# A routing stage rewritten: slot table by float16 products, probabilities after it, counts ahead of the prefix product, last gate by halves

## The reference

```
logits = einsum('bsd,de->bse', x, w_gate)
local_gate = 1 / (1 + exp(-einsum('bsd,de->bse', x, w_local)))
for b, s:
    fresh_e = argmax(logits[b, s])
    e = fresh_e if s == 0 or local_gate[b, s] < 0.5 else prev_e
    prev_e = e
    p = softmax(logits[b, s])            # the sum has 1e-9 added
    h = relu(x[b, s] @ w1[e])            # 512 -> 1024
    out[b, s] = p[e] * (h @ w2[e])       # 1024 -> 512
```

## Time and profile before

| | |
|---|---|
| median of three runs | 1024.58 us (1024.54 to 1025.24) |
| the profiled execution's own time | 1025.83 us |
| its span from the first to the last instruction | 1023.7 us |
| busy in the span: PE, DVE, ACT, POOL | 92%, 45%, 35%, 25% |
| the last tile's second product ends | at 665.4 us |
| first product of the expert blocks starts | at 711.0 us |

### The profile page before, as it was taken

One profiled execution on the slowest core, in us unless ns is written; L12 is line 12 of the kernel. 1 busy time (PEld: TensorE's weight loads), 2 busy tenths in 40 slices (PEclk: granted clock), 3 DMA queues, 4 the chain that ended last, 5 costly groups with the idle time before them and its releaser, 6 DMA issues.

```text
span 1023.7 us, 20276 instructions
## 1 busy us (share of the span) xinstructions
PE 940.4 (92%) x7890; PEld 613.2 (60%) x7891; DVE 458.1 (45%) x830; ACT 356.0 (35%) x472; POOL 254.1 (25%) x265
## 2 busy tenths in 40 slices
PE   4899997999999999999999999915899999999995
PEld 2566665787767677676777676603455555555552
DVE  4688885465334242433333343558924786000000
ACT  2677774443111111121221111010444454454442
POOL 2345543110101010110202000001334444334331
PEclk9999998999999999999999999956899999999998
DMA  8243441433101110101101102403734664111100
GB/s 300 83 137 122 138 125 40 137 104 118 55 28 35 41 41 20 41 20 41 41 20 41 41 11 98 139 23 131 234 91 162 197 210 150 41 38 40 46 25 1
DMA packets 50812, 87.18 MB, mean 85 GB/s; under 512 B 6069, under 2 KB 21636, under 8 KB 50510
## 3 DMA queue, kind: packets, MB, share of 16 engines
q1 hardware_dynamic: 45325, 70.52, 21.6%
q0 software_dynamic: 5440, 16.00, 5.0%
HBM read 71.78 MB, written 16.55 MB: 86 GB/s over the span
## 4 chain that ended last, share of the span: by engine, by line
PE 86%; DVE 8%; issue 2%; DMA 1%; ACT 1%; POOL 1%; DVEq 0%; SPq 0%; POOLq 0%; ACTq 0%
PE psum L743 18%; PE psum L758 18%; PE psum L891 13%; PE psum L867 12%; PE psum L688 6%; PE psum L543 5%; PE psum L700 2%; PE psum L880 2%; DVE m_mem L1146 2%; DVE arena L1174 2%; PE psum L855 1%; PE psum L564 1%; PE psum L598 1%; PE psum L617 1%; PE psum L718 1%
## 5 line engine op out<-in xcount | busy, mean ns | idle before, releaser
L743 PE MATMUL psum<-m_mem,arena 128*128 (+1 forms) x1728 | 198.8, 273 | 0.3 <-DVE arena L1376 0.3
L758 PE MATMUL psum<-arena,m_mem 128*128 128x512 f16 x864 | 195.3, 379 | 0.0
L743 PEld LDWEIGHTS psum<-m_mem,arena 128*128 128x128 f16 x1728 | 168.3, 98 | 26.0 <-DVE arena L1376 0.6
L758 PEld LDWEIGHTS psum<-arena,m_mem 128*128 128x128 f16 x864 | 84.5, 98 | 90.4
L867 PE MATMUL psum<-arena,m_mem 128*128 x600 | 137.0, 386 | 1.4 <-ACT m_mem L1077 1.4
L891 PE MATMUL psum<-arena,m_mem 128*128 x600 | 133.6, 379 | 2.3 <-ACT m_mem L1091 2.3
L1022 ACT ACTIVATE m_mem<-psum 128x512 f16<-128x512 f32 x72 | 43.0, 597 | 257.8 <-PE psum L743 255.8
L867 PEld LDWEIGHTS psum<-arena,m_mem 128*128 128x128 f16 x600 | 58.7, 99 | 69.0 <-issue 5.9
L1292 DVE SCALAR_TENSOR_TENSOR m_mem<-psum,m_mem 128x512 f16<-128x512 f32 x72 | 49.8, 691 | 111.6 <-ACT m_mem L1022 109.6
L891 PEld LDWEIGHTS psum<-arena,m_mem 128*128 128x128 f16 x600 | 57.7, 98 | 67.5 <-issue 2.4
L1574 POOL TENSOR_TENSOR arena<-m_mem,arena 128x1024 f16<-128x1024 f32 x9 | 17.9, 1994 | 264.7 <-ACT arena L1032 264.7
(11 more groups left out here) (198 smaller groups left out, 1147.8 us busy)
## 6 DMA issues: line engine op xcount, KB each, us to landing
dimdft_sb<-in_exp_w SPq DMA_DIRECT2D x74, 256.0 KB, 3.2
wstage<-in_exp_w SPq DMA_DIRECT2D x54, 256.0 KB, 2.8
m_mem<-in_qk SPq DMA_DIRECT2D x16, 576.0 KB, 4.7
arena<-in_v SPq DMA_DIRECT2D x32, 160.0 KB, 4.3
x_rows<-m_mem SPq DMA_DIRECT2D x16, 320.0 KB, 3.1
x_rows<-arena SPq DMA_DIRECT2D x9, 512.0 KB, 2.8
wstage<-in_mlp_w SPq DMA_DIRECT2D x16, 256.0 KB, 2.7
arena<-in_mlp_w SPq DMA_DIRECT2D x16, 256.0 KB, 2.7
```

What stands on the lines that cost most here:

```text
L743: last = nc.tensor.matmul(psum[:, 2 + k % 4, (f % 2) * 2 * P:(f % 2 + 1) * 2 * P], w1_sb[:, sp_, c, f * P:(f + 1) * P], unT[:, bass.ds(t % ...
L758: last = nc.tensor.matmul(psum[:, 6 + q, :], hT[:, k % 4, sp_, at:at + P], w2_sb[:, mp, f, :], start=f == 0 and sp_ == 0 and mp == 0, stop ...
```

## The change

Four edits.

1. **Last gate by halves.** Behind the last tile, the 256 rows go through transpose, high part, low part and gate in two halves of 128 rows, each with its own semaphore. `x2_done` is now raised by DVE behind the second low part. DVE also subtracts one prefix matrix from the other there.
2. **Running counts ahead.** `onehot` is made directly from PSUM, and DVE scans it along the groups (`ocum`) before the product. The product of the triangle less the ones with `onehot`, plus that of the ones with `ocum`, gives the position within the expert; an extra product of 8 columns gives the totals. The copies to `ef`, `tot` and the two additions into `before` are gone, and `psel` runs behind the scan.
3. **Slots on partitions, in float16.** `onehot_slot` becomes the weights, in float16, and `row_vals` (row number less 1152) the moving side with 25 columns, so the table's first column comes out in place. Its one consumer, the gather of block 0, starts from it directly, without POOL's copy. 
4. **The rest afterwards.** The expert of each block, the three bfloat16 parts of the probability (`p_part`, `p_vals`), the tokens (`tok_vals`), and 36 more products on PE follow behind `table_ready`, and the other table columns, seven small instructions, behind those (`rest_ready`). On PE the 36 products stand ahead of `transpose_xe(0)`. Four small DVE instructions (a float16 copy of the place numbers, the offset ids) are added where DVE waits for the DRAM transfer.

```diff
@@ end of the last tile, PE
-            transpose_x2(MT - 1)
-            gate(MT - 1)
+            for q in range(2):
+                pe.wait_ge(end_x2, q + 1)
+                for c in range(DC):
+                    last = nc.tensor.transpose(psum[:, q, c * P:(c + 1) * P], x2_sb[:, q, c * P:(c + 1) * P],
+                                               ident_sb[:, :])
+                last.then_inc(end_turned, 1)
+            for q in range(2):
+                pe.wait_ge(end_lo, q + 1)
+                last = gate_half(q)
+            last.then_inc(gate_ready, 1)
@@ end of the last tile, ACT
-            x2T_copy(MT - 1)
+            for q in range(2):
+                act.wait_ge(end_turned, q + 1)
+                nc.scalar.activation(x2T[:, 0, q], psum[:, q, :], ACT.Copy).then_inc(end_hi, 1)
             x2_hi_of(MT - 1)
@@ end of the last tile, DVE
-            x2T_lo_of(MT - 1)
+            x2_of(MT - 1, False, end=True)
+            dve.wait_ge(tables_in, 9 * 16)
+            nc.vector.tensor_tensor(prefix_sb[:, 0, :], prefix_sb[:, 0, :], prefix_sb[:, 1, :], ALU.subtract)\
+                .then_inc(parts_ready, 1)
+            for q in range(2):
+                dve.wait_ge(end_hi, q + 1)
+                nc.vector.tensor_tensor(x2T[:, 1, q], psum[:, q, :], x2T[:, 0, q], ALU.subtract).then_inc(end_lo, 1)
+            dve.wait_ge(end_x2, 2)
+            dve.sem_inc(x2_done, 1)
             logits_of(MT - 1)
@@ counts and slot table, PE
-            nc.tensor.matmul(psum[:, 3, 0:E * NT], prefix_sb[:, 1, :], flat1h, start=True, stop=True)
-            nc.tensor.matmul(psum[:, 4, 0:E * NT], prefix_sb[:, 0, :], flat1h, start=True, stop=True)\
+            pe.wait_ge(parts_ready, 1)
+            nc.tensor.matmul(psum[:, 4, 0:E * NT], prefix_sb[:, 0, :], flat1h, start=True, stop=False)
+            pe.wait_ge(onehot_ready, 2)
+            nc.tensor.matmul(psum[:, 3, 0:E], prefix_sb[:, 1, :], ocum[:, :, NT - 1], start=True, stop=True)
+            nc.tensor.matmul(psum[:, 4, 0:E * NT], prefix_sb[:, 1, :], ocum.rearrange("p e n -> p (e n)"), start=False, stop=True)\
                 .then_inc(counts_ready, 1)
             for n in range(NT):
                 pe.wait_ge(rec_ready, n + 2)
-                last = nc.tensor.matmul(psum[0:3 * NBLK, 5, 0:P], slot_vals[:, n].rearrange("p w k -> p (w k)"),
-                                        onehot_slot[:, n, :], start=n == 0, stop=n == NT - 1)
+                last = nc.tensor.matmul(psum[:, 5, 0:NBLK], onehot_slot[:, n, :], row_vals[:, n, :],
+                                        start=n == 0, stop=n == NT - 1)
             last.then_inc(slots_ready, 1)
-            pe.wait_ge(slots_copied, 1)
-            nc.tensor.transpose(psum[:, 6, 0:3 * NBLK], slotsT[0:3 * NBLK, :], ident_sb[0:3 * NBLK, 0:3 * NBLK])\
-                .then_inc(slots_ready, 1)
+            pe.wait_ge(vals_ready, 1)
+            for n in range(NT):
+                nc.tensor.matmul(psum[:, 1, 0:NBLK], onehot_slot[:, n, :], tok_vals[:, n, :],
+                                 start=n == 0, stop=n == NT - 1)
+                last = nc.tensor.matmul(psum[:, 7, 0:3 * NBLK], onehot_slot[:, n, :],
+                                        p_vals[:, n].rearrange("p w k -> p (w k)"), start=n == 0, stop=n == NT - 1)
+            last.then_inc(slots_ready, 1)
@@ counts, DVE
-            step(nc.vector.tensor_copy(ef, psum[:, 2, 0:NT]))
-            step(nc.vector.tensor_tensor(onehot, iota_sb, bc(ef, E, 1), ALU.is_equal))
-            nc.vector.tensor_tensor(psel, onehot, pex.rearrange("p n e -> p e n"), ALU.mult)\
+            nc.vector.tensor_tensor(onehot, iota_sb, bc(psum[:, 2, 0:NT], E, 1), ALU.is_equal).then_inc(onehot_ready, 1)
+            dve.wait_ge(onehot_ready, 1)
+            nc.vector.tensor_tensor_scan(fl(ocum), fl(reset_sb), fl(onehot), 0.0, ALU.mult, ALU.add)\
                 .then_inc(onehot_ready, 1)
+            step(nc.vector.tensor_tensor(psel, onehot, pex.rearrange("p n e -> p e n"), ALU.mult))
             dve.wait_ge(counts_ready, 1)
-            step(nc.vector.tensor_copy(tot, psum[:, 3, 0:E * NT].rearrange("p (e n) -> p e n", e=E)))
-            step(nc.vector.tensor_tensor_scan(fl(run), fl(reset_sb), fl(tot), 0.0, ALU.mult, ALU.add))
-            step(nc.vector.tensor_tensor(over, bc(run[:, :, NT - 1], NT, 2), thr_sb, ALU.is_gt))
+            step(nc.vector.tensor_tensor(over, bc(psum[:, 3, 0:E], NT, 2), thr_sb, ALU.is_gt))
...
-            step(nc.vector.tensor_tensor(before, run, tot, ALU.subtract))
-            step(nc.vector.tensor_tensor(before, before, bc(start, NT, 2), ALU.add))
@@ slot table, DVE
-            step(nc.vector.tensor_copy(posf2, posi))
-            nc.vector.tensor_reduce(psl, psel.rearrange("p e n -> p n e"), AX.X, ALU.add)
-            step(nc.vector.tensor_tensor(isblk, blk_iota, bc(posf2[:, 1, :], NBLK, 2), ALU.is_equal))
-            nc.vector.tensor_tensor(slot_vals[:, :, 0, :], isblk, bc(ids_sb[:, 0, :], NBLK, 2), ALU.mult)
-            nc.vector.tensor_tensor(slot_vals[:, :, 1, :], isblk, bc(ids_sb[:, 1, :], NBLK, 2), ALU.mult)
-            nc.vector.tensor_tensor(slot_vals[:, :, 2, :], isblk, bc(psl, NBLK, 2), ALU.mult).then_inc(rec_ready, 1)
+            nc.vector.tensor_copy(posf2, posi[:, 0, :])
+            step(nc.vector.tensor_tensor(isblk, blk_iota, bc(posi[:, 1, :], NBLK, 2), ALU.is_equal))
+            nc.vector.tensor_tensor(row_vals, isblk, bc(id_vals[:, 0, :], NBLK, 2), ALU.mult).then_inc(rec_ready, 1)
             for n in range(NT):
-                nc.vector.tensor_scalar(onehot_slot[:, n, :], slot_iota, posf2[:, 0, n:n + 1], None, ALU.is_equal)\
+                nc.vector.tensor_scalar(onehot_slot[:, n, :], iota_h, posf2[:, n:n + 1], None, ALU.is_equal)\
                     .then_inc(rec_ready, 1)
+            step(nc.vector.tensor_reduce(psl, psel.rearrange("p e n -> p n e"), AX.X, ALU.add))
+            dve.wait_ge(slots_ready, 1)
+            nc.vector.tensor_scalar(table[:, :, 0], psum[:, 5, 0:NBLK], float(MID), None, ALU.add).then_inc(table_ready, 1)
...
+            step(nc.vector.tensor_copy(p_part[:, 0, :], psl))
+            step(nc.vector.tensor_tensor(p_rest[:, 0, :], psl, p_part[:, 0, :], ALU.subtract))
+            step(nc.vector.tensor_copy(p_part[:, 1, :], p_rest[:, 0, :]))
+            step(nc.vector.tensor_tensor(p_rest[:, 1, :], p_rest[:, 0, :], p_part[:, 1, :], ALU.subtract))
+            step(nc.vector.tensor_copy(p_part[:, 2, :], p_rest[:, 1, :]))
+            for w in range(3):
+                nc.vector.tensor_tensor(p_vals[:, :, w, :], isblk, bc(p_part[:, w, :], NBLK, 2), ALU.mult)
+            nc.vector.tensor_tensor(tok_vals, isblk, bc(id_vals[:, 1, :], NBLK, 2), ALU.mult).then_inc(vals_ready, 1)
             dve.wait_ge(slots_ready, 2)
...
+            nc.vector.tensor_tensor(table[:, :, 2].bitcast(F32), psum12, psum[:, 7, 2 * NBLK:3 * NBLK], ALU.add)\
+                .then_inc(rest_ready, 1)
@@ POOL
+                if first:
+                    index = table[:, 0, 0:1]
+                else:
+                    index = inrec[:, 0:1]
...
             gather_block(0, first=True)
             gather_block(1)
+            pool.wait_ge(rest_ready, 1)
             set_outrec(0, first=True)
```

More of the change, by code:

```diff
@@ L65 @@
 RING = 2 + SPARE
+MID = TOK // 2
 ONES = 19
@@ L279, in fused_kernel @@
         assert place["at"] <= tables_at
-        place["at"] = seq_at
-        isblk = carve([NT, NBLK], F32)
         place["at"] = seq_at
@@ L395, in fused_kernel @@
         table_ready = sem("table_ready")
+        rest_ready = sem("rest_ready")
         inrec_set = sem("inrec_set")
@@ L720, in transpose_x2, with gate_half @@
                 last.then_inc(x2T_ready, 1)
+            def gate_half(q):
+                for c in range(DC):
+                    for sp_, mp in THREE:
+                        last = nc.tensor.matmul(psum[:, 0, q * (E + 1):(q + 1) * (E + 1)],
+                                                x2T[:, sp_, q, c * P:(c + 1) * P], wg_sb[:, mp, c, :],
+                                                start=c == 0 and sp_ == 0 and mp == 0,
+                                                stop=c == DC - 1 and sp_ == 1)
+                return last
             def gate(t):
@@ L725, in gate @@
                 for q in range(2):
-                    for c in range(DC):
-                        for sp_, mp in THREE:
-                            last = nc.tensor.matmul(psum[:, 0, q * (E + 1):(q + 1) * (E + 1)],
-                                                    x2T[:, sp_, q, c * P:(c + 1) * P], wg_sb[:, mp, c, :],
-                                                    start=c == 0 and sp_ == 0 and mp == 0,
-                                                    stop=c == DC - 1 and sp_ == 1)
+                    last = gate_half(q)
                 last.then_inc(gate_ready, 1)
@@ L1294, in hidden_lo, with x2_of @@
                     .then_inc(h_lo, 1)
-            def x2_of(t, first):
```

(14 more changed lines are left out.)

72 lines of the change are left out of this document (46 added, 26 removed).

## The result

The changed kernel takes 1017.59 us (median of 4 runs, 1016.08 to 1018.81) against 1024.56 us for the kernel before on the same chip: 0.9931 of it, with an interval of 0.9914 to 0.9949, so some 7.0 us less (5.2 to 8.8). I had said 1016.7 with a range of 1014.2 to 1019.4. The profiled execution took 1018.81 us, its span is 1016.8 against 1023.7.

The account below looks back on a forecast made before the run. PE was taken to bound the expert blocks, so an earlier start moves the end. Terms 0.5 + 1.65 + 6.6 - 1.05 + 0.2 = 7.9 us gave 1024.58 - 7.9 = 1016.7 us, range 1014.2 to 1019.4.

Parts of the forecast that it names:

- What bounds the kernel: Expert blocks: PE bounds them from 730 us on, busy 281.6 of 294 us, so an earlier start moves the end.
- Part 1: Last tile's gate by halves: 0.5 us gained, bounds 0.3 and 1.8, since POOL's low part holds DVE's routing up.
- Part 2: Running counts, from the chosen experts' arrival to `posi`: copies and additions leave the chain, 1.65 us gained (1.4 to 1.8).
- Part 3: Slot table, from `posi` to `table_ready`: float16 one-hot tables with slots on partitions, 6.6 us gained (6.0 to 7.7).
- Part 4: From `table_ready` to block 0's transposes: values, then 36 products, take 6.9 us against 5.86, 1.05 us lost.
- one of my signs, that the gather has landed while PE waits for `vals_ready`: Ahead of block 0's transposes: gather lands 4.2 us behind `table_ready`, values come at 4.4, transposes directly follow the 36 products.
- the 6 to 8 that I had set: From `table_ready` to block 0's transposes: under 6 or over 8 us would show the prediction wrong.
- The clock: PE's granted clock around up(0): 2.5 us more PE work ahead may raise it sooner, 0.2 us gained.
- the later products weigh: 36 products before block 0 at L841's pace (7.1 for 2.5 us), broadcasts at 0.75: 1021.9 us, chance 0.10.
- the gather comes late: Block 0's gather, with POOL waiting for DVE, lands 7.8 us behind `table_ready`: 1017.6 us, chance 0.06.
- the halves pay in full: Last tile's gate: POOL's low part does not hold DVE up, 1.8 us gained there: 1015.4 us, chance 0.10.
- The one that ends slower: First blocks: lower clock holds, a 24-product group takes 10.4 instead of 5.18 us; 1027.1 us with two groups, chance 0.03.

Follow-up runs that it names:

- the run with fills: Changed kernel with unread products in PE's waits (11, 4, 16 and 9, from the later values to the last down product): 1013.19 us, 0.9882 of the kernel before.

## Why the prediction was right, step by step

- **What bounds the kernel: right.** The blocks follow PE, 11.70 us each in every kernel, and what the front gains arrives in them. DVE stayed ahead; nothing was given back between the first and the last block.
- **Part 1: 0.5 taken, 0.65 measured.** POOL's low part does hold DVE, as L1410's 0.68 had said; the halves are worth 1.73 only where the stall is gone. The Trainium skill ("SBUF — State Buffer", "SBUF: two separate sides") says that a DVE instruction in a two-port mode or with two SBUF inputs and a GpSimd instruction shut each other out for a whole instruction, whichever came first; the traces agree, with 1.77 us for L1455 beside POOL and 0.18 without it. L1455 has one SBUF input, and the profile doesn't say in which mode it ran. Not in the sum is the way from the end of that instruction to the first one behind both exchanges through DRAM, 13.57 us after and 13.35 before: 0.2 back.
- **Part 2: 1.65 taken, 1.72 measured** (5.92 to 4.20), and as much by the run that undoes it.
- **Part 3: 6.6 taken, 6.69 measured** (11.55 to 4.86). The one-hot tables started every 0.163 us for my 0.17, and took 3.01 for 3.15. I had said nothing of whether type or orientation brings it; the type does.
- **Part 4: 1.05 lost by the sum, 0.24 measured.** `vals_ready` came 4.4 us behind `table_ready`, as worked out, broadcasts at 0.54 a start for my 0.60. The term that was mis-sized is the 36 products: 2.5 us by the estimate, from the first at 698.28 to the transposes' start 1.63. In the timeline a pair starts every 0.091 us, not every 0.14; with PE's clock up in the run with fills it is 0.060. I had doubled a price of the full clock; at these few columns the pace did not double. The other misread size is the gather. I had it 4.2 us behind `table_ready`, ahead of the values and 2.7 us too early. It landed 4.0 us behind its issue in the run with the products moved, 4.77 behind `table_ready` and so later than the values (4.41): the transposes could start only 1.3 us earlier, and one of my signs, that the gather has landed while PE waits for `vals_ready`, is not borne out. From `table_ready` to the transposes it took 6.10 us, just inside the 6 to 8 that I had set.
- **The clock: the step that failed.** I took 0.2 gained, because PE would have worked 2.5 us more ahead of up(0). That looked at the 36 later products alone. Part 3 also takes 7.10 us of float32 passes away and puts 2.96 us in their place, so PE's work from the slot table to up(0) fell from 8.4 to 5.6 us, and "PE's work ahead of up(0) only grows" is wrong. up(0) took 1.05 us more, not less, and up(1) gave 1.4 back: over the two, 0.35 was gained, close to my 0.2 but by luck. What my sum had no term for is the last down product, 7.04 us for 5.35, 1.69 lost, and POOL's low part of block 0 beside DVE's splits (2.66 for 2.17), 0.5 lost. Of the 8.58 us gained at up(0) that leaves 8.58 - 1.05 - 0.5 + 1.4 - 1.69 = 6.74, so 1.8 were lost where I had added 0.2. Two errors partly cover each other: part 4 was 0.8 better than said and this term 2.0 worse, so the sum's 7.9 became 6.9. The forecast's own range, 1015 to 1018.8, held the time; that it lies so near the middle is in part that luck.
- **The rivals.** That the later products weigh is refuted (1.63 us for 7.1). That the gather comes late is refuted: its issue took 0.97 beside DVE's two-input work, and in the run with the later products moved it landed 4.77 us behind `table_ready` and not 7.8. That the halves pay in full is true of the gate alone, not of this kernel. The one that ends slower, a low clock held for two blocks, named the clock but not the place: the first two up products together took 0.35 us less than before, and the 1.69 lost lie in the last down product.

up(0) and up(1) together, beyond 5.34 each, cost 3.5 us before (1.51 and 1.95), 3.1 after (2.56 and 0.55), and between 2.9 and 4.2 in every other profile without fills ahead of them; with the fills, nothing. So within the first blocks the change only moved this loss from one product to the next, and the fills removed it.

The last down product goes with up(1). Of the nine profiles in which its wait is not filled, it took 7.04 us in the five whose up(1) took 5.9 to 6.1 (the changed kernel twice, float32, part 2 undone, the gate whole without the stall), and 5.35 in the four whose up(1) took 7.1 to 7.5 (the kernel before, POOL's low part late, the later products behind the transposes, the gate whole). So some 1.3 us less at up(1) came each time with 1.7 more at the end. In the run with only the last wait filled, up(1) took 6.1 and the last product still 5.34, which speaks for the fill. These are nine executions and no mechanism: whether the change or the execution decides between the two kinds stays open. So does what raises the clock ahead of up(0): 36 float32 passes had it rise in the kernel before, and in the run with float32 tables it stayed at 0.50 through 7.89 us of them and 5.4 us into up(0).

## What to carry to other kernels

Take a routing stage apart by distances from one event that the change does not touch: 1.7 us showed clearly there in one profile while the total's spread of 5 us hid it. Before a chain on DVE is shortened, look which instruction of another engine will then lie over it; here the shortened chain brought 0.65 us, and moving one GpSimd instruction out of its way another 1.6. Where a clock term enters a sum, count all the work that the change takes away from PE, and look at the last product as well as at the first. Where PE waits a few microseconds ahead of long products, look at their duration: products that nobody reads took 5 us out of a kernel whose other stages stayed as they were.

## What the runs showed of the hardware

- At a granted clock of 0.50 a float32 pass started every 0.213 us, with 128 weight columns and 25 moving ones (run with float32 tables) as with 75 and 128 (kernel before); at 1.00 the latter started every 0.11. In float16, 18 products with 128 weight and 25 moving columns kept up with tables that started every 0.163 us, at 0.50.
- Pairs of float16 and bfloat16 products of 25 and 75 moving columns, each with its own 128 weight columns, started every 0.091 us at a granted clock of 0.50 and every 0.060 at 1.00.
- DVE and POOL held each other up both ways: 18 elements on DVE took 1.77 us beside POOL and a split of 0.42 us took 2.34, and POOL's low part took 2.66 beside DVE's splits, 2.12 to 2.17 in other blocks.
- A semaphore raised by DVE on its own passed an instruction still running on that engine: ACT, which waited for it, started 0.62 us before that instruction's end.
- Broadcasts of 450 elements that read and write float16 took 0.62 us, as long as those that read float32 (L1512): the 16-bit type gave nothing there.
